# Local attention feeding a gated expert on one core: the first chunk's attention in buffers of its own, its rows of x loaded first, low parts of the weights on TensorE, loops written out, transposes a step closer

## The chip, the core and the metric

One core of one Trainium2 chip runs the program. The metric is the device time of one execution in microseconds (us), the median of several runs. A profile is one further execution, recorded by the hardware.

## What is computed

`x` is [4, 4160, 192]; `weight_gen` holds 8 heads x 7 taps per token. Each token's row is a softmax-weighted sum of the 7 rows that end at it. That goes through an expert with a hidden width of 1024, whose gate is a 3-tap convolution along the sequence:

```python
w = softmax(weight_gen, axis=-1)                     # [B, S, 8, 7]
x_unf = x_pad[:, idx, :].reshape(B, S, K, H, group)  # 7 rows that end at s
a = einsum('bshk,bskhg->bshg', w, x_unf).reshape(B, S, D)
h = maximum(a @ w_in, 0)                             # [B, S, 1024]
conv_out = sum(conv_w[k] * hp[:, k:k + S, :] for k in range(3))
gate = 1 / (1 + exp(-conv_out))
out = (h * gate) @ w_out                             # [B, S, 192]
```

## The kernel before, in words

**Chunks and steps.** The 16,640 tokens are cut into 20 chunks of 832. A chunk passes through 8 steps, one for each 128 of the 1024 hidden columns (j = 0 to 7). Every engine has its own instruction stream and runs the same sequence of steps `step(it, k)`, each with its part of the work; semaphores tie the streams together. `pipeline` writes steps 0 to 31 out, runs five rounds of a hardware loop (`Fori`) over 24 steps (three chunks, since buffers are rings of three), and writes the last 33 out.

**Attention of a chunk** (120 partitions, each with 7 tokens and the 13 rows of x they need). SyncE (SP) loads `x_win`, `logits` and `mask`. VectorE (DVE) takes maxima; GpSimd (POOL) or DVE subtracts them; ScalarE (ACT) takes exponentials; DVE sums and inverts; POOL multiplies by the inverse and by the mask into `soft` (L266, L272). Then, for i = 0 to 6: POOL multiplies the seven rows by `soft` into `weighted` (`product`, L280; a ring of three buffers, so product n waits for sum n - 3), and DVE adds up the taps into `attn` (`sum_taps`, L588). Products 2 and 5 of the first chunk are DVE's (`SHARED`). TensorE (PE) transposes `attn` in four rounds (`ROUNDS`, `turn`, L711) into the one bank `turn_ps`; ACT copies each round out as the high part (`take_turned`, L494, L496), and DVE subtracts for the low part (`low_part`, L596, L600). A round can start only when the low part of the round before has been read off the bank.

**The expert.** In each step PE multiplies the split activations by the split weights into `z` (L686, ten matmuls of 418 columns, two for each of five pairs of parts; `z` is a ring of three), two steps ahead of DVE. ACT applies relu into `hidden` (L460) and the centre tap (L467), DVE the outer taps (L558, L564), ACT the sigmoid (L478). The product with `hidden` is POOL's for six of eight steps (L417) and DVE's for j = 2 and 5 (L570). A finished output tile of 128 tokens is eight fp32 products with `wo` (L700, the trace shows each as two instructions); ACT copies it out (L503), SP stores it. A tile belongs to a step: steps 0 to 5 of the first of three chunks have one, and steps 0 to 6 of the other two; the last one or two steps of a chunk have none. The first tile is in step 32, where all of chunk 0 must be gated.

**What sets the order.** `attention_at` places the attention of chunk c at step 24 + 8c - LEAD plus a slot: maxima at -9, exponentials at -6, sums at 0 to 6, and the rounds of transposes at 4, 6, 8 and 10. LEAD is 14. POOL works two steps ahead (AHEAD) on attention, and its first chunk's products are at steps 8 to 14. In a step, PE does `product_in`, then the output tile, then `turn`.

**The start.** SP issues logits of chunks 0 and 1, the mask, x of chunk 0 (row 0 apart, then 119 partitions in one DMA, L334), the weights into `stage_a` and `stage_b` (which lie in `gated`), `wo`, and the 3072 convolution weights one by one (L386). ACT rounds the weights to their high parts (L508, L509); DVE subtracts for the low parts `wa_lo`, `wb_lo` (`weights_low`, L547), in its stream between two sums of the first chunk.

Of the kernel before, what the change touches and what calls it, by code (L numbers as in the profile page):

```python
# [11 lines left out]
P = 128  # L12
# [3 lines left out]
LEAD = 14  # L16
AHEAD = 2
LOAD = -8
LOAD_W = -10
SHARED = (2, 5)  # L20
# [28 lines left out]
def local_attention_gated_expert(nc, x, weight_gen, w_in, conv_w, w_out, masks, out):  # L49
# [18 lines left out]
    EARLY = 5  # L68
    ON_DVE = J - len(POOL_STEPS)
# [9 lines left out]
    def chunk_at(it, step):  # L79

        d, j = divmod(step, J)
        if isinstance(it, int) and not 0 <= RING * it + d < NC:
            return None
        return Chunk(it, d), j
# [8 lines left out]
    def tile_at(it, k):  # L93

        turn, step = divmod(k - J, RING * J)
# [18 lines left out]
    def products(c, i):  # L114

        first = isinstance(c.number, int) and c.number == 0
        return c.number * GROUP + i + 1 - len([n for n in SHARED if n <= i or not first])

    def attention_at(it, k, slot):

        found = chunk_at(it, k + LEAD - slot)
        return found[0] if found and found[1] == 0 else None
# [6 lines left out]
    def pipeline(eng, step):  # L129
# [3 lines left out]
        for k in range(0, 32):  # L133
            step(-1, k)
        with nc.Fori(0, 5, engines=(eng.engine,), hint_back_edge=True) as it:
            for k in range(8, 32):
                step(it, k)
        for k in range(8, 41):
            step(5, k)

    with ExitStack() as ctx:
# [43 lines left out]
        s_ident = sem("s_ident")  # L185
        s_weights_hi = sem("s_weights_hi")
# [33 lines left out]
        ROUNDS = [(4, False, 0, MID), (6, True, 0, MID), (8, False, MID, GROUP), (10, True, MID, GROUP)]  # L220
# [11 lines left out]
        def turned(i0, i1):  # L232

            return turn_ps[:, 0:(i1 - i0) * PA].rearrange("p (i c) -> p c i", c=PA)
# [5 lines left out]
        def x_landed(c):  # L240

            value = 16 * (c.turn + 1) + (16 if c.ring == 0 else 0)
# [8 lines left out]
        def shared(c, i):  # L251

            return first(c) and i in SHARED

# [19 lines left out]
        def multiply(engine, c, i):  # L274
# [4 lines left out]
            y = weighted[0:PA, (c.ring * GROUP + i) % RING, :].rearrange("p (h g k) -> p k h g", h=H, k=K)  # L279
# [10 lines left out]
        def softmax_at(it, k, slot):  # L290
# [4 lines left out]
            if c and single(c):  # L295
                return [(Chunk(0, d), 1, slice(d % RING, d % RING + 1)) for d in (c.number, c.number + 1)] \
                    if c.number % 2 == 0 else []
# [8 lines left out]
        def logits_landed(c, count):  # L306


            if single(c):
                return s_logits[c.number], 32 if c.number == 0 else 16  # L310
# [5 lines left out]
        def _(sp):  # L316
            def load(c):
                base = c.number * CHUNK
                if not isinstance(c.number, int) or c.number >= RING:

                    sp.wait_ge(s_weighted, (c.number - RING + 1) * GROUP - len(SHARED))
                    if isinstance(c.number, int) and c.number == RING:
                        sp.wait_ge(s_weighted_dve, len(SHARED))
                start = 1 if first(c) else 0
# [4 lines left out]
                if first(c):  # L329

                    sp.wait_ge(s_cleared, 2)
                    sp.dma_start(x_win[0:1, c.ring, K * D:], x_flat[0:K - 1, :].rearrange("(o a) b -> o (a b)", o=1)) \
                        .then_inc(s_x[c.ring], 16)
                sp.dma_start(x_win[start:end, c.ring, :],  # L334
                             bass.AP(x_flat.tensor, (base - K + GROUP * start) * D,
                                     [[GROUP * D, end - start], [1, WIN * D]])).then_inc(s_x[c.ring], 16)
# [7 lines left out]
            def load_logits(c, count):  # L344

                wait(sp, s_soft, c.number - (RING - 1 if single(c) else 0))
                landed = logits_landed(c, count)[0]
                for d in range(count):
                    chunk = Chunk(c.turn, c.ring + d)
                    start = 1 if first(chunk) else 0  # L350
                    end = PA - 1 if isinstance(c.number, int) and chunk.number == LAST else PA
                    if start:

                        sp.wait_ge(s_cleared, 1)
                        sp.dma_start(logits[0:1, 0, HK:], w_flat[0:GROUP - 1, :].rearrange("(o a) b -> o (a b)", o=1)) \
                            .then_inc(landed, 16)
                    sp.dma_start(logits[start:end, chunk.ring, :],
                                 bass.AP(w_flat.tensor, (chunk.number * CHUNK - 1 + GROUP * start) * HK,
                                         [[GROUP * HK, end - start], [1, GROUP * HK]])).then_inc(landed, 16)
# [7 lines left out]
            def step(it, k):  # L367
                for c, count, _ in softmax_at(it, k, LOAD_W):
                    load_logits(c, count)
                c = attention_at(it, k, LOAD)  # L370
                if c:
# [5 lines left out]

            k0 = J * RING - LEAD + J + LOAD_W
            for k in range(0, k0 + 1):
# [3 lines left out]
            sp.dma_start(stage_b[D2:P, :], w_in[P:D, :]).then_inc(s_weights, 16)  # L383
            sp.dma_start(wo[:, :, :], w_out.rearrange("(j p) d -> p j d", p=P)).then_inc(s_weights_out, 16)
            with nc.allow_non_contiguous_dma("3072 convolution weights, once"):
                sp.dma_start(cw[:, :, :], conv_w.rearrange("t (j p) -> p t j", p=P)).then_inc(s_weights_out, 16)  # L386
            for k in range(k0 + 1, 32):
                step(-1, k)
            with nc.Fori(0, 5, engines=(sp.engine,), hint_back_edge=True) as it:
# [402 lines left out]
```

## Time and profile before

| | |
|---|---|
| runs (3) | median 788.49 us, 787.89 to 789.17 |
| profiled execution | 786.22 us, span 784.4 us in the profile |
| PE busy | 701.6 us, 89% of the span |
| DVE busy | 675.3 us, 86% |
| POOL busy | 611.4 us, 78% |
| ACT busy | 523.9 us, 67% |
| granted TensorE clock, mean | 0.993 of full |
| chain that ended last | PE 81%, DVE 8%, ACT 4%, issue 3%, DMA 2% |

The span runs from the first recorded instruction to the last; the execution's own time is 1.8 us longer. "The chain" follows the last instruction back to whatever released each step. A "wait" is idle time of an engine, put down to the event that ended it.

### The profile page before, as it was taken

The page shows a single profiled execution, that of the slowest core. Times are in us where ns is not written, and L with a number is a line of the kernel's source. Part 1 is how long each engine was busy: PE and PEld are TensorE (multiplying, and loading weights), DVE is VectorE, ACT ScalarE, POOL GpSimd, SP SyncE. Part 2 cuts the span into 40 slices and gives each one's busy share as a digit, 9 for nine tenths or more (in the row PEclk, how much of TensorE's full clock was granted, in tenths as well). Part 3 has the DMA queues.
Part 4 walks back from the last instruction along what each step waited for, and adds up shares of the span by engine and source line. Part 5 has one row for each costly group of instructions (what it writes and reads, how often), then busy time and mean ns, then how long its engine had stood idle before and what let it go on. Part 6 is the DMA issues. An engine that isn't in the chain of part 4 may idle for free.

```text
span 784.4 us, 12158 instructions
## 1 busy us (share of the span) xinstructions
PE 701.6 (89%) x4008; PEld 672.9 (86%) x4008; DVE 675.3 (86%) x648; ACT 523.9 (67%) x719; POOL 611.4 (78%) x308
## 2 busy tenths in 40 slices
PE   0116698999999999989999899999999998999998
PEld 0016598999999999989999899999999998999998
DVE  3898999898999898998989998989989898985650
ACT  1117678676687676786667876678767678676761
POOL 1889999888888888998879888889878888852320
PEclk9999799999999999999999999999999999999999
DMA  7820130303323031303124030313123030000001
GB/s 155 173 54 1 30 78 16 83 21 82 78 51 72 20 82 38 91 15 83 48 50 107 21 77 20 82 41 82 42 55 79 24 90 18 20 16 21 18 26 36
DMA packets 31292, 43.11 MB, mean 55 GB/s; under 512 B 8551, under 2 KB 28614, under 8 KB 28872
## 3 DMA queue, kind: packets, MB, share of 16 engines
q1 hardware_dynamic: 31270, 42.82, 22.0%
q8 instruction: 13, 0.21, 0.1%
q14 instruction: 9, 0.07, 0.0%
HBM read 30.03 MB, written 12.78 MB: 55 GB/s over the span
## 4 chain that ended last, share of the span: by engine, by line
PE 81%; DVE 8%; ACT 4%; issue 3%; DMA 2%; POOL 1%; SPq 0%; ACTq 0%; DVEq 0%; POOLq 0%
PE out_ps L700 42%; PE z L686 34%; DVE attn L588 3%; PE turn_ps L711 3%; DMA x_win<-in_x 2%; PE z L742 2%; DVE z L558 1%; POOL weighted L280 1%; ACT hidden L460 1%; ACT L478 1%; ACT gated L478 1%; DVE z L564 1%; DVE weighted L280 1%; ACT xa_hi L496 0%; DVE wb_lo L547 0%
## 5 line engine op out<-in xcount | busy, mean ns | idle before, releaser
L280 POOL TENSOR_TENSOR weighted<-x_win,soft 120x1344 f32<-120x1344 f32 x138 | 380.7, 2768 | 55.4 <-DVE attn L588 44.2
L700 PE MATMUL out_ps<-wo,gated 128*128 128x192 f32 x2016 | 352.4, 328 | 8.1 <-ACT out_sb L503 8.1
L700 PEld LDWEIGHTS out_ps<-wo,gated 128*128 128x128 f32 x2016 | 327.6, 187 | 22.7 <-ACT out_sb L503 15.4
L417 POOL TENSOR_TENSOR gated<-gated,hidden 128x832 f32<-128x832 f32 x119 | 197.9, 1663 | 87.4 <-ACT gated L478 87.4
L588 DVE TENSOR_REDUCE attn<-weighted 120x192 f32<-120x1344 f32 x140 | 215.9, 1545 | 5.3 <-POOL weighted L280 3.3
L460 ACT ACTIVATE hidden<-z 128x836 f32<-128x836 f32 x160 | 138.7, 867 | 100.7 <-PE z L686 92.0
L558 DVE SCALAR_TENSOR_TENSOR z<-hidden,cw,z 128x832 f32<-128x832 f32 x160 | 173.1, 1082 | 16.4 <-ACT z L467 15.2
L564 DVE SCALAR_TENSOR_TENSOR z<-hidden,cw,z 128x832 f32<-128x832 f32 x160 | 174.0, 1088 | 4.3
L467 ACT ACTIVATE z<-hidden,cw 128x832 f32<-128x832 f32 x160 | 153.4, 959 | 5.2
L686 PE MATMUL z<-xa_hi,wa_hi 128*128 128x418 f32 x320 | 103.5, 405 | 20.8 <-ACT gated L478 9.3
L478 ACT ACTIVATE gated<-z 128x832 f32<-128x832 f32 x119 | 102.4, 861 | 27.0 <-DVE z L564 25.8
L711 PE MATMUL turn_ps<-ident,attn 120*128 120x120 f32 x280 | 44.1, 275 | 50.9 <-DVE attn L588 34.7
L686 PE MATMUL z<-xa_hi,wa_lo 128*128 128x418 f32 x320 | 88.3, 357 | 0.0
L686 PE MATMUL z<-xa_lo,wa_hi 128*128 128x418 f32 x320 | 88.3, 357 | 0.0
L686 PE MATMUL z<-xb,wb_hi 128*128 128x418 f32 x320 | 87.9, 356 | 0.0
L686 PE MATMUL z<-xb,wb_lo 128*128 128x418 f32 x320 | 87.8, 356 | 0.0
L711 PEld LDWEIGHTS turn_ps<-ident,attn 120*128 120x128 f32 x280 | 35.5, 146 | 55.2 <-issue 44.3
L686 PEld LDWEIGHTS z<-xa_hi,wa_hi 128*128 128x128 f32 x320 | 52.4, 192 | 26.5 <-ACT gated L478 12.8
L686 PEld LDWEIGHTS z<-xb,wb_hi 128*128 128x128 f32 x320 | 61.3, 192 | 1.0
L686 PEld LDWEIGHTS z<-xa_hi,wa_lo 128*128 128x128 f32 x320 | 61.2, 191 | 1.0
L686 PEld LDWEIGHTS z<-xa_lo,wa_hi 128*128 128x128 f32 x320 | 61.3, 192 | 0.8
L686 PEld LDWEIGHTS z<-xb,wb_lo 128*128 128x128 f32 x320 | 61.1, 191 | 0.6
(43 smaller groups left out, 378.2 us busy)
## 6 DMA issues: line engine op xcount, KB each, us to landing
x_win<-in_x SPq DMA_DIRECT2D x18, 1170.0 KB, 7.9
out<-out_sb SPq DMA_DIRECT2D x127, 96.0 KB, 1.6
logits<-in_weight_gen SPq DMA_DIRECT2D x18, 183.8 KB, 9.0
x_win<-in_x SPq DMA_DIRECT2D x2, 1160.2 KB
wo<-in_moe_w_out SPq DMA_DIRECT2D x1, 768.0 KB, 15.9
gated<-in_moe_w_in SPq DMA_DIRECT2D x1, 512.0 KB, 5.6
gated<-in_moe_w_in SPq DMA_DIRECT2D x2, 256.0 KB, 16.4
mask<-in_masks SPq DMA_DIRECT2D x20, 23.0 KB, 1.7
```

Of the source, the lines that this page charges most:

```text
L280: return engine.tensor_tensor(y, rows, s, ALU.mult)
L417: nc.gpsimd.tensor_tensor(to, to, hidden[:, (c.ring * J + j) % RING, 1:1 + CHUNK], ALU.mult) \
L460: nc.scalar.activation(hidden[:, r, :].rearrange("p (a b) -> p a b", a=2), both(r, HALF), ACT.Relu).then_inc(s_hidden, 1)
L467: nc.scalar.activation(both(r, OH), hidden[:, r, 1:1 + CHUNK].rearrange("p (a b) -> p a b", a=2), ACT.Copy, scale=cw[:, 1, j:j + 1]).then_ ...
L478: nc.scalar.activation(to, both(r, OH), ACT.Sigmoid).then_inc(s_gate, 1)
L558: nc.vector.scalar_tensor_tensor(out=both(r), in0=halves(hidden[:, r, 0:CHUNK]), scalar=cw[:, 0, j:j + 1], in1=both(r), op0=ALU.mult, op1= ...
L564: nc.vector.scalar_tensor_tensor(out=both(r), in0=halves(hidden[:, r, 2:2 + CHUNK]), scalar=cw[:, 2, j:j + 1], in1=both(r), op0=ALU.mult, ...
L588: nc.vector.tensor_reduce(attn[0:PA, i, :], y, AX.X, ALU.add).then_inc(s_attn, 1)
L686: last = nc.tensor.matmul(z[r][:, half, 0:HALF], weights, moving[:, half * HALF:(half + 1) * HALF], start=(m == 0), stop=(m == len(parts) ...
L700: last = nc.tensor.matmul(out_ps[0:end - u * P, 0:D], gated[:, j, u * P:end], wo[:, j, :], start=(j == 0), stop=(j == J - 1))
L711: last = nc.tensor.transpose(turn_ps[:, (i - i0) * PA:(i - i0 + 1) * PA], src, ident[0:PA, 0:PA])
L742: last = nc.tensor.matmul(bank[0:end - u * P, 0:D], gated[:, j, u * P:end], wo[:, j, :], start=(j == 0), stop=(j == J - 1))
```

## The change

- **First chunk.** It leaves the common sequence: SP issues `load_first`, POOL its six products, DVE `attention_first`, PE and ACT its four rounds, all before `pipeline`. Its products go to `gated[:, i, ...]`, a buffer for each i, and its rounds to four banks (`FIRST_BANKS`), so neither waits for a buffer. Only product 2 is DVE's. The maxima of chunk 1 move behind two sums.
- **Loads.** x of chunk 0 and its logits are cut into 112 and 7 partitions; x goes ahead of logits 1 to 3 and of the weights, the mask of chunk 0 behind x. The convolution weights come as 24 rows and are transposed on PE.
- **Low parts of the weights** come from PE: the staged weight times the identity, plus the high part times minus the identity, in PSUM, copied out by ACT.
- **Order.** LEAD is 13; the rounds are at slots 4, 6, 7 and 9, so rounds 3 and 4 keep their steps and all else of attention is a step later. PE does `turn` ahead of the output tile. POOL normalises the next chunk straight behind product 6.
- **Loops.** All 185 steps are written out.

The diff, cut to its core:

```diff
-LEAD = 14
+LEAD = 13
-SHARED = (2, 5)
+BY_VECTOR = 2
+    EVEN = 1 + PA // 16 * 16
-        for k in range(0, 32):
-            step(-1, k)
-        with nc.Fori(0, 5, engines=(eng.engine,), hint_back_edge=True) as it:
-            for k in range(8, 32):
-                step(it, k)
-        for k in range(8, 41):
-            step(5, k)
+        for k in range(STEPS):
+            step(-1, k)
-        ROUNDS = [(4, False, 0, MID), (6, True, 0, MID), (8, False, MID, GROUP), (10, True, MID, GROUP)]
+        ROUNDS = [(4, False, 0, MID), (6, True, 0, MID), (7, False, MID, GROUP), (9, True, MID, GROUP)]
+        FIRST_BANKS = [turn_ps, out_ps, z[2][:, 0, :], z[2][:, 1, :]]
+            y = by_hand(i) if first(c) else weighted[:, (c.ring * GROUP + i) % RING, :]
...
+            def load_first():
+                for a, b in ((1, EVEN), (EVEN, PA)):
+                    sp.dma_start(logits[a:b, 0, :], ...)
+                sp.wait_ge(s_cleared, 1)
+                sp.dma_start(logits[0:1, 0, HK:], ...)
+                for a, b in ((1, EVEN), (EVEN, PA)):
+                    sp.dma_start(x_win[a:b, 0, :], ...)
+                sp.wait_ge(s_cleared, 2)
+                sp.dma_start(x_win[0:1, 0, K * D:], ...)
+                sp.dma_start(mask[0:PA, 0, :], ...)
...
+            def normalise_next(c):
+                pool.wait_ge(s_weighted, products(c, GROUP - 1))
+                if first(c):
+                    pool.wait_ge(s_weighted_dve, 1)
+                normalise(pool, nc.gpsimd, Chunk(0, c.number + 1))
...
-            def weights_low():
-                for part, (hi, lo, stage) in enumerate(((wa_hi, wa_lo, stage_a), (wb_hi, wb_lo, stage_b))):
-                    dve.wait_ge(s_weights_hi, part + 1)
-                    nc.vector.tensor_tensor(lo[:, :], stage, hi[:, :].bitcast(F32), ALU.subtract)
+            def attention_first():
+                softmax_begin(c); sums(c); reciprocals(c); normalise(dve, nc.vector, c)
+                first_product(c, BY_VECTOR)
+                sum_taps(c, 2); sum_taps(c, 0); softmax_begin(after)
+                sum_taps(c, 1); sum_taps(c, 3); sums(after); reciprocals(after)
+                sum_taps(c, 4); low_part(c, 0); sum_taps(c, 5); low_part(c, 1)
+                sum_taps(c, 6); low_part(c, 2); low_part(c, 3)
...
+            exponent(Chunk(0, 0), 1, slice(0, 1))
+            split_weights()
+            exponent(Chunk(0, 1), 1, slice(1, 2))
+            take_conv_weights()
+            take_turned(Chunk(0, 0), 0)
+            take_rest()
+            for r in range(1, len(ROUNDS)):
+                take_turned(Chunk(0, 0), r)
...
+            def rest_of_weights():
+                pe.wait_ge(s_minus, 1)
+                for part, (hi, stage) in enumerate(((wa_hi, stage_a), (wb_hi, stage_b))):
+                    pe.wait_ge(s_weights_hi, part + 1)
+                    for half in range(2):
+                        f = slice(half * F // 2, (half + 1) * F // 2)
+                        nc.tensor.matmul(z[part][:, half, :], ident[:, :], stage[:, f], start=True, stop=False)
+                        last = nc.tensor.matmul(z[part][:, half, :], minus, hi[:, f], start=False, stop=True)
+                    last.then_inc(s_rest, 1)
```

Three places where rows stand in another order now.

**SP, from the start of its stream** (names are the tiles written and the inputs read). Before:

```order
L355 DMA logits<-in_weight_gen 1x336
L357 DMA logits<-in_weight_gen 119x392
L357 DMA logits<-in_weight_gen 120x392
L326 DMA mask<-in_masks 120x49
L332 DMA x_win<-in_x 1x1152
L334 DMA x_win<-in_x 119x2496
L381 DMA gated<-in_moe_w_in 128x1024
L382 DMA gated<-in_moe_w_in 64x1024
L383 DMA gated<-in_moe_w_in 64x1024
```

Now:

```order
L368 DMA logits<-in_weight_gen 112x392
L368 DMA logits<-in_weight_gen 7x392
L372 DMA logits<-in_weight_gen 1x336
L375 DMA x_win<-in_x 112x2496
L375 DMA x_win<-in_x 7x2496
L379 DMA x_win<-in_x 1x1152
L381 DMA mask<-in_masks 120x49
L361 DMA logits<-in_weight_gen 120x392
L404 DMA gated<-in_moe_w_in 128x1024
```

x stands ahead of the mask and of the logits of chunk 1, as 112 and 7 partitions in place of 119.

**POOL, the first two chunks** (`gated` here is the first chunk's product buffer). Before, from the product that starts chunk 0:

```order
L280 TENSOR_TENSOR weighted<-x_win,soft 120x7x192 [waits s_x0,s_soft]
L280 TENSOR_TENSOR weighted<-x_win,soft 120x7x192
L280 TENSOR_TENSOR weighted<-x_win,soft 120x7x192 [waits s_attn] x3
L266 TENSOR_TENSOR soft<-expo,inverse 120x7x8x7 [waits s_inverse,s_weighted_dve,s_weighted]
L272 TENSOR_TENSOR soft<-soft,mask 120x392 [waits s_mask1,s_norm]
L280 TENSOR_TENSOR weighted<-x_win,soft 120x7x192 [waits s_attn,s_x1,s_soft]
L280 TENSOR_TENSOR weighted<-x_win,soft 120x7x192 [waits s_attn] x6
```

Now:

```order
L295 TENSOR_TENSOR gated<-x_win,soft 120x7x192 [waits s_x0,s_soft]
L295 TENSOR_TENSOR gated<-x_win,soft 120x7x192 x5
L280 TENSOR_TENSOR soft<-expo,inverse 120x7x8x7 [waits s_inverse,s_weighted_dve,s_weighted]
L286 TENSOR_TENSOR soft<-soft,mask 120x392 [waits s_mask1,s_norm]
L295 TENSOR_TENSOR weighted<-x_win,soft 120x7x192 [waits s_x1,s_soft]
L295 TENSOR_TENSOR weighted<-x_win,soft 120x7x192 x2
L295 TENSOR_TENSOR weighted<-x_win,soft 120x7x192 [waits s_attn] x4
```

Six products stand in place of five, none of them with a wait for a sum; of chunk 1's seven, the first three have none.

**ACT, around the exponentials of three chunks**, once in 24 steps. Before (the copies to `out_sb` are the output tiles; the first one here is the fourth of its 24 steps):

```order
L503 COPY out_sb<-out_ps 128x192
L481 REGISTER_ALU
L484 ACT_TABLE_LOAD
L484 ACTIVATE expo<-logits 120x168x7
L454 REGISTER_ALU
L459 REGISTER_ALU
L460 ACTIVATE hidden<-z 128x836
L467 ACTIVATE z<-hidden,cw 128x2x416
L491 REGISTER_ALU
L494 CAST xb<-turn_ps 64x120x3
L478 ACT_TABLE_LOAD
```

Now, behind the fifth copy:

```order
L521 CAST xb<-turn_ps 64x120x3
L505 ACTIVATE z<-z 128x2x416
L530 COPY out_sb<-out_ps 128x192
L511 ACT_TABLE_LOAD
L511 ACTIVATE expo<-logits 120x168x7
L487 ACTIVATE hidden<-z 128x836
L494 ACTIVATE z<-hidden,cw 128x2x416
L505 ACT_TABLE_LOAD
```

The exponentials and the second table load moved a step later, behind the last round's copy (`xb`), to where one more tile of the chunk follows and then two steps without a tile.

## Rows read from the trace of the kernel before

**Rows 1.** Busy time by stretch: window, length, busy of PE, PEld, DVE, ACT, POOL, clock, DMA.

```profile
0.00:57.27 57.27, 3.73 (x14) 2.38 (x15) 41.66 (x41) 7.71 (x11) 33.27 (x20) 1.00 0.60 131
57.27:99.14 41.87, 29.28 (x129) 26.69 (x129) 38.86 (x39) 28.52 (x34) 39.63 (x21) 0.88 0.05 14
99.14:700.00 600.86, 587.16 (x3395) 564.86 (x3395) 552.46 (x530) 440.15 (x604) 518.61 (x257) 1.00 0.22 55
```

**Rows 2.** PE's waits from 110 to 700 us: total us, times, longest.

```profile
PE out_ps L700 <- ACT out_sb L503: 8.1, 7, 1.4
PE z L686 <- ACT gated L478: 5.6, 6, 0.9
```

**Rows 3.** The chain that ended last, at the start: start us, us, what.

```profile
2.79 15.73 DMA x_win<-in_x
...
57.27 3.43 PE z L686 x10
```

**Rows 4.** Timeline of POOL: start, us, line, out<-in, count, idle before it.

```profile
18.66 12.28 POOL L280 TENSOR_TENSOR weighted<-x_win,soft 120x1344 f32<-120x1344 f32 x4 [11.11 <-DMA x_win<-in_x]
34.67 2.65 POOL L280 TENSOR_TENSOR weighted<-x_win,soft 120x1344 f32<-120x1344 f32 x1 [3.74 <-DVE attn L588]
37.40 0.91 POOL L266 TENSOR_TENSOR soft<-expo,inverse 120x392 f32<-120x392 f32 x1
...
39.33 9.44 POOL L280 TENSOR_TENSOR weighted<-x_win,soft 120x1344 f32<-120x1344 f32 x3
51.70 10.27 POOL L280 TENSOR_TENSOR weighted<-x_win,soft 120x1344 f32<-120x1344 f32 x4 [2.93 <-DVE attn L588]
...
97.14 1.66 POOL L417 TENSOR_TENSOR gated<-gated,hidden 128x832 f32<-128x832 f32 x1 [0.84 <-ACT gated L478]
```

**Rows 5.** Loads of x, all of them: from issue to landing.

```profile
DMA to landing us min/median/max: 7.6/7.9/14.0
```

**Rows 6.** DMA traffic in two stretches; the last two columns are DMA share and GB/s.

```profile
5.00:10.00 5.00, 0.00 (x0) 0.00 (x0) 4.70 (x9) 1.06 (x2) 0.87 (x1) 1.00 1.01 218
15.40:16.80 1.40, 0.00 (x0) 0.00 (x0) 0.00 (x0) 0.00 (x0) 0.00 (x0) 1.00 0.40 125
```

**Rows 7.** Timeline of DVE at the start.

```profile
8.81 0.57 DVE L272 TENSOR_TENSOR soft<-soft,mask 120x392 f32<-120x392 f32 x1
...
18.62 2.56 DVE L280 TENSOR_TENSOR weighted<-x_win,soft 120x1344 f32<-120x1344 f32 x1 [8.17 <-DMA x_win<-in_x]
...
39.46 3.42 DVE L547 TENSOR_TENSOR wa_lo<-gated,wa_hi 128x1024 fp32r<-128x1024 f32 x1
...
47.61 1.47 DVE L259 TENSOR_TENSOR logits<-logits,top 120x392 f32<-120x392 f32 x1
```

**Rows 8.** Line L280: duration min/median/max ns, first and last start.

```profile
L280 POOL TENSOR_TENSOR weighted<-x_win,soft x138: 2587/2746/4872, 18.7 to 688.8; 120x1344 f32<-120x1344 f32 x138
```

**Rows 9.** The page's groups: busy, mean ns of one, idle before.

```profile
L417 POOL TENSOR_TENSOR gated<-gated,hidden 128x832 f32<-128x832 f32 x119 | 197.9, 1663 | 87.4 <-ACT gated L478 87.4
L460 ACT ACTIVATE hidden<-z 128x836 f32<-128x836 f32 x160 | 138.7, 867 | 100.7 <-PE z L686 92.0
...
L467 ACT ACTIVATE z<-hidden,cw 128x832 f32<-128x832 f32 x160 | 153.4, 959 | 5.2
...
L478 ACT ACTIVATE gated<-z 128x832 f32<-128x832 f32 x119 | 102.4, 861 | 27.0 <-DVE z L564 25.8
```

**Rows 10.** Timeline of PE: the first output tile, and one round of 24 steps.

```profile
99.14 2.76 PE L700 MATMUL out_ps<-wo,gated 128*128 128x192 f32 x16
...
230.43 2.87 PE L700 MATMUL out_ps<-wo,gated 128*128 128x192 f32 x16 [1.11 <-ACT out_sb L503]
...
238.46 0.65 PE L686 MATMUL z<-xa_hi,wa_hi 128*128 128x418 f32 x2 [0.94 <-ACT gated L478]
```

**Rows 11.** Timeline of ACT in the same round.

```profile
223.12 1.28 ACT L484 ACT_TABLE_LOAD   x1
224.41 1.19 ACT L484 ACTIVATE expo<-logits 120x1176 f32<-120x1176 f32 x1
```

More of the change, by code:

```diff
@@ L114, in products @@
     def products(c, i):
-        first = isinstance(c.number, int) and c.number == 0
-        return c.number * GROUP + i + 1 - len([n for n in SHARED if n <= i or not first])
+        return c.number * GROUP + i + 1 - (1 if c.number > 0 or i >= BY_VECTOR else 0)
     def attention_at(it, k, slot):
-        found = chunk_at(it, k + LEAD - slot)
-        return found[0] if found and found[1] == 0 else None
+        for c in range(1, NC):
+            if k == J * RING + c * J - LEAD + STALL + slot:
+                return Chunk(0, c)
+        return None
     def wait(eng, sem, value):
@@ L319, in load @@
                 if not isinstance(c.number, int) or c.number >= RING:
[L321 to L324, printed above, removed]
+                    sp.wait_ge(s_weighted, products(Chunk(0, c.number - RING), GROUP - 1))
+                    if c.number == RING:
+                        sp.wait_ge(s_weighted_dve, 1)
                 end = PA - 1 if isinstance(c.number, int) and c.number == LAST else PA
@@ L368, in step @@
                 for c, count, _ in softmax_at(it, k, LOAD_W):
-                    load_logits(c, count)
+                    if not single(c):
+                        load_logits(c, count)
                 c = attention_at(it, k, LOAD)
-                if c:
+                if c and c.number >= RING:
                     load(c)
@@ L375, in step @@
                     store(*found)
-            k0 = J * RING - LEAD + J + LOAD_W
-            for k in range(0, k0 + 1):
-                step(-1, k)
+            load_first()
+            load_logits(Chunk(0, 1), 1)
             sp.dma_start(stage_a, w_in[0:P, :]).then_inc(s_weights, 16)
@@ L383, in _ @@
             sp.dma_start(stage_b[D2:P, :], w_in[P:D, :]).then_inc(s_weights, 16)
+            sp.dma_start(conv_rows, conv_w.rearrange("t (j p) -> (t j) p", p=P)).then_inc(s_conv_rows, 16)
+            load_logits(Chunk(0, 2), 1)
+            load_logits(Chunk(0, 3), 1)
+            load(Chunk(0, 1))
             sp.dma_start(wo[:, :, :], w_out.rearrange("(j p) d -> p j d", p=P)).then_inc(s_weights_out, 16)
[L385 to L389, printed above, removed]
-                for k in range(8, 32):
-                    step(it, k)
-            for k in range(8, 41):
-                step(5, k)
+            load(Chunk(0, 2))
+            pipeline(step)
             for turn, u in last_tiles():
@@ L442, in step @@
                     apply_gate(*found)
-            pipeline(pool, step)
+            for i in range(GROUP):
+                if i != BY_VECTOR:
+                    product(Chunk(0, 0), i)
+            normalise_next(Chunk(0, 0))
+            pipeline(step)
         @block.scalar
```

204 lines of the change are left out of this document (127 added, 77 removed).

## The prediction

> **What bounds the kernel now.** I read the stretches first. From 99.14 us, where the first output tile starts, to 700 us PE is busy 587.2 of 600.9 us, DVE 552.5, POOL 518.6 [rows 1]. So from the first tile on PE alone sets the time, and the end is the start of that tile plus 784.4 - 99.1 = 685.3 us. Ahead of it PE did little: 3.7 of 57.3 us, then 29.3 of 41.9. PE's waits give the rest: 13.7 us from 110 to 700, all of it for ACT (8.1 for copies of output tiles, 5.6 for sigmoids), and none without a named cause [rows 2]. The chain of waits shows what held the start: 15.7 us for x of chunk 0, and z of chunk 0 only at 57.27 [rows 3]. The timeline of POOL then shows a nearly full engine up to the last gate of chunk 0 at 98.8 us, 0.3 us ahead of the first tile [rows 4, 10]. So the change is worth what it takes off POOL's chain up to that gate, plus what it does to the 13.7 us.
>
> **Part 1: when the first product starts.** Before, x was issued at 2.79 and landed at 18.52 [rows 3]; product 0 started at 18.66 [rows 4]. In the last of that transfer only 0.40 of the DMA engines' time was used, at 125 GB/s; from 5 to 10 us it was all of it, at 218 [rows 6]. The 120-partition loads of x land in 7.6 to 7.9 us, the largest value being 14.0 [rows 5]. So 119 partitions are the odd case, not the size.
>
> The Trainium skill (DMA: Bandwidth & Descriptors, "Why a DMA increments its semaphore by 16 and not by 1") says that a DMA is spread over the largest number of engines, up to 16, that divides its outer dimension: 119 gives 7, 112 gives 16. The share of 0.40 agrees (7/16 is 0.44). By the rule 112 partitions go in seven rounds where 120 take eight on 15, so x would land an eighth sooner than 7.6 us, about 1 us less than what I take.
>
> Now x is issued behind three DMAs of logits, at some 2.0 us. At the landing time of a 120-partition load it would be there at 9.6 to 9.9; the seven partitions, row 0 and the mask come behind it in the same queue. I take 10.6 for the last of them, and DVE's multiplication by the mask, 0.57 us [rows 7], which used to be done long ahead and now waits for it. The first product starts at **11.2**. Low bound 10.2 (nothing behind x costs anything), high bound 16.6 (14.0 us for x).
>
> **Part 2: POOL's chain to the last gate of chunk 0.** Product 0 starts together with DVE's product, as before, and takes the longest time of the line, 4.87 us, which is DVE's 2.56 and then its own [rows 7, 8]. Five more have no wait and no other two-operand work of DVE beside most of them: 2.6 each (shortest 2.587 [rows 8]), to 11.2 + 4.9 + 13.0 = 29.1. Normalising chunk 1 takes from 37.40 to 39.33, 1.9 [rows 4]: 31.0. Seven products of chunk 1 at 10.27/4 = 2.57 [rows 4]: 49.0. Chunk 2 is normalised: 50.9. Then seven products of chunk 2 at the median 2.75 [rows 8], another normalisation and six gates at 1.66 [rows 9]: 19.2 + 1.9 + 10.0, to 82.0. Before, the stretch from 61.97 to 98.80 held the same and one product more, which LEAD 13 moves behind the gate: 35.8 of work in 36.8, so 1.0 idle. I keep it: 83.0.
>
> What went, against 18.66: POOL's two waits for a sum, 3.74 and 2.93 [rows 4], which came of the ring of three buffers and of the low parts in DVE's stream (3.42 and its twin [rows 7]); 0.5 us on each of three products beside these (9.44/3 against 2.57 [rows 4]); one product. What came: one product for POOL in place of DVE (2.6, counted).
>
> What could be late next is DVE and PE. The low parts on PE are four fp32 and four split matmuls of 512 columns. Eight fp32 products of 192 columns take 2.76 us at the full clock [rows 10], so 512 columns cost about 0.9, or 1.8 at 1.2 GHz; a split matmul of 418 columns took 0.34 us when z of chunk 0 came out of a pause [rows 3], so 512 cost 0.42. That is 4 x 2.2 = 8.9 us at the low clock. It starts when the weights are in and rounded: 1 MB behind x at 218 GB/s [rows 6] is 16, with the first cast some 17.5 us. PE is free between 24 and 26.4, where round 1 of the transposes could start at about 23.5 (fourth sum); ACT then copies both low parts ahead of round 2. DVE ends the last low part at 33.6 to 35.4, does the maxima and subtractions of chunks 2 and 3 (each subtraction 0.6 to 1.5 [rows 7]) and the first sum of chunk 1 by 38.4 to 40.5. POOL's fourth product of chunk 1 needs that sum and is due at 31.0 + 7.7 = 38.7. So 0 to 2 us of wait; I take 1. The gate ends at 84.0, the first tile starts at **84.3** against 99.14: **14.8 us** less.
>
> The Trainium skill (SBUF — State Buffer, "SBUF: two separate sides") says that DVE with two SBUF inputs and POOL exclude each other for a whole instruction. The rows above agree (4.87 is one behind the other). By the rule each of DVE's three subtractions in this stretch could wait out a whole product, 2.6 us, where the row of this trace shows 1.47 in place of about 0.6; the wait of POOL would then be 4 us, not 1.
>
> From the taps on DVE is close behind POOL as before: between first tap and first tile it has seven sums, eight pairs of taps, and one low part more than it had (0.66). It stays some 2 us ahead of the last gate by my count, so it costs nothing; if POOL is faster than I think, DVE is the next bound, at about 82.
>
> **Part 3: from the first tile on.** PE's work is the same. The loops' back edges go; PE had no unexplained idle [rows 2], so this is worth 0. POOL enters with one product less done (2.7 us), at 518.6/600.9 = 86% load [rows 1]; the first chunk with tiles may stall for part of it: **+1**.
>
> The ACT waits: once in 24 steps ACT loads a table, takes exponentials (1.28 + 1.19 [rows 11]) and loads a table again; PE then waits 1.11 + 0.94 = 2.05 us [rows 10], first for the copy of a tile, then for a sigmoid. The exponentials now come one step later, behind one more tile copy and the copy of the last transposes. By the timeline of that round: PE finishes the next tile without waiting, since the copy ahead of it is done; then come the two steps without a tile, where z needs sigmoids one and two steps back. The next tile's copy would be done at some 227.8; table and exponentials end at 230.3; relu 0.87, centre tap 0.96, table 1.28 and sigmoid 0.86 [rows 9, 11] give the first sigmoid at 234.3, and copy, relu, tap and sigmoid the next at 237.3. PE, with a tile and two z between, would ask at 233.7 and 236.6: 1.3 us in place of 2.05. Over six to seven rounds that is nearly 5; I take **-3**, since DVE may be late for a sigmoid. Bounds: all of the 13.7 us goes, or each round pays 2.05 more, +12.
>
> Rounds 1 to 2 and 2 to 3 of the transposes are now two and one steps apart. Round 3 needs DVE's low part of round 2, issued in the same step. PE spends some 4.5 us in a step with a tile; from the end of z to that low part I count 7.4 us over two such steps, against 9.4 until PE asks for it. It costs nothing as long as the margin of 2 us holds. All else that moves (SP's loads, turns ahead of tiles) keeps its distance.
>
> **Sum.** -14.8 + 1 - 3 = **-16.8 us**. The profiled execution took 786.22 (span 784.4 and 1.8 around it): 769.4. It lay 2.27 below the median of the runs, so the median becomes 788.49 - 16.8 = **771.7 us**.
>
> **The rivals.**
> 1. *The start is later than that* (chance 0.2): x lands late, PE runs the low parts at the low clock throughout, and DVE's subtractions wait out whole products, so POOL waits 4 or more. For: nothing of this overlap was in the trace. Against: POOL's chain was tight before too. 2 to 8 us more: 774 to 780.
> 2. *ACT's waits all but vanish* (0.13): the step without a tile absorbs the table loads. For: they were only 2.05 a round. Against: my timeline still finds two. 7 to 10 us less than the forecast, 762 to 765.
> 3. *Slower* (0.03): the rounds bind. If round 3 waits w us for the low part of round 2 in every chunk after the first, it costs 19w. The gain of 16.8 is gone from w = 0.9; at w = 2 the time is 788.5 - 16.8 + 38 = 810. For: DVE is at 92% [rows 1], so it fills 4.1 of the 4.5 us of a step. Against: the 2 us of margin above.
> 4. *It doesn't do what it says* (0.04): PE gets its first tile 15 us sooner but DVE, not PE, sets the pace for the rest, so the lead is paid back: 786 to 789. Against: DVE's 92% [rows 1] leaves 48 us of slack.
>
> The forecast itself has 0.60. **The range** is 762 to 780: it takes in rivals 1 and 2 for the greater part, and the bounds on the first product (-1, +5) and on ACT. A difference of 0.2% is 1.6 us, about what a measurement of this kernel can tell from none. **Faster 0.95, same 0.01, slower 0.04** (rival 3 and a share of rival 4).
>
> **What would show it.** In the profile after: first product of POOL near 11 us; its chunk 0 products in one piece of about 18 us without a wait; z of chunk 0 near 34 to 36; first tap near 46; first tile near 84; PE's waits for ACT after that 9 to 11 us in all, with none for transposes. A first tile after 88, a total of waits above 16, or a row of PE waiting for L640 or L644 in each chunk would make the prediction wrong.

## The result, and the profile after

The changed kernel takes **766.61 us** (median of 4 runs, 765.41 to 767.54) against 788.19 for the kernel before on the same chip (786.99 to 789.17): a ratio of 0.9729, 95% interval 0.9709 to 0.9749, or 21.6 us less. I had forecast 16.8 less. It is inside the range, but the parts do not fall where I put them. The profiled execution took 767.54 us with a span of 765.8, 18.7 less than that of the kernel before (786.22), which lay at the low end of its runs while this one lies at the high end. (Two of the four executions took 765.4 and 765.8 us, two 767.4 and 767.5; the profiled one is the longest.)

The page of the changed kernel, busy time and the slices of PE:

```profile
PE 707.7 (92%) x4021; PEld 681.8 (89%) x4021; DVE 666.6 (87%) x646; ACT 526.1 (69%) x723; POOL 610.6 (80%) x308
...
PE   1655899999999999999999999999999999999998
```

Busy time by stretch, columns as in [rows 1]; the cuts are the first z of chunk 0 and the first output tile:

```profile
0.00:33.11 33.11, 9.26 (x28) 5.33 (x28) 23.09 (x31) 8.84 (x13) 22.56 (x15) 0.93 0.92 211
33.11:86.04 52.93, 32.43 (x128) 28.82 (x129) 49.84 (x45) 29.45 (x35) 47.81 (x25) 0.79 0.08 20
86.04:700.00 613.96, 603.19 (x3501) 586.65 (x3502) 565.55 (x544) 454.21 (x626) 526.92 (x262) 1.00 0.22 55
```

The first z starts at 33.11 and the first tile at 86.04, against 57.27 and 99.14 [rows 1, 3]: of the 24 us won at z, 11 are gone by the first tile, since DVE and POOL need 52.9 us for what lies between, where they needed 41.9 with more of chunk 1 already done. From the first tile to the end the span is 765.8 - 86.04 = 679.8 us, against 685.3. So 13.1 us came ahead of the first tile and 5.5 behind it.

The start, on POOL, DVE and PE, in that order. The rows answer to [rows 4, 7, 10]:

```profile
11.02 17.70 POOL L295 TENSOR_TENSOR gated<-x_win,soft 120x1344 f32<-120x1344 f32 x6 [9.55 <-DVE soft L286]
...
30.73 8.02 POOL L295 TENSOR_TENSOR weighted<-x_win,soft 120x1344 f32<-120x1344 f32 x3
40.58 10.20 POOL L295 TENSOR_TENSOR weighted<-x_win,soft 120x1344 f32<-120x1344 f32 x4 [1.83 <-DVE attn L631]
```

```profile
10.37 0.57 DVE L286 TENSOR_TENSOR soft<-soft,mask 120x392 f32<-120x392 f32 x1 [3.24 <-DMA mask<-in_masks]
...
33.59 2.60 DVE L273 TENSOR_TENSOR logits<-logits,top 120x392 f32<-120x392 f32 x1
36.11 0.55 DVE L650 TENSOR_REDUCE top<-logits 120x56 f32<-120x392 f32 x1
36.69 2.34 DVE L273 TENSOR_TENSOR logits<-logits,top 120x392 f32<-120x392 f32 x1
```

```profile
23.58 0.57 PE L776 MATMUL turn_ps<-ident,attn 120*128 120x120 f32 x4
...
86.04 4.52 PE L763 MATMUL out_ps<-wo,gated 128*128 128x192 f32 x16 [2.04 <-POOL gated L445]
```

Product 0 starts at 11.02 (forecast 11.2), the six products take 17.70 us in one piece (17.9), and POOL waits once, 1.83 us, for the first sum of chunk 1. That sum is late because each of DVE's two subtractions took about as long as a product of POOL. PE waited 2.04 us for POOL's last gate, and then ran its first tile in 4.52 us in place of 2.76; the granted clock of the stretch is 0.71:

```profile
86.04:92.00 5.96, 5.96 (x25) 5.94 (x26) 5.22 (x6) 4.28 (x7) 5.96 (x3) 0.71 0.04 12
```

PE's waits from 110 to 700 us answer to [rows 2] (`issue` stands where the profile names nothing that ended the wait):

```profile
PE out_ps L763 <- issue: 6.1, 6, 1.6
PE z L749 <- ACT gated L505: 4.6, 11, 0.7
```

They sum to 10.7 us against 13.7. In a period of 24 steps they are 0.3 us shorter (1.78 against 2.05 [rows 10]), yet the period takes 105.3 us (the tile that waits starts at 122.62, 227.89, 333.18) where it took 106.2 (124.17, 230.43, 336.64). A part of what was won behind the first tile stands in no wait at all. That was the question for the experiments, beside what each part of the start is worth.

### The profile page after: what moved, and what is told of

It reads as the page before. It is cut to its first block, busy times and chain, and to the rows that moved or that the text cites. A ratio compares the mean times of both kernels' runs of the same rounds, so it can differ in the third digit from the quotient of the medians.

```text
span 765.8 us, 10644 instructions
## 1 busy us (share of the span) xinstructions
PE 707.7 (92%) x4021; PEld 681.8 (89%) x4021; DVE 666.6 (87%) x646; ACT 526.1 (69%) x723; POOL 610.6 (80%) x308
## 4 chain that ended last, share of the span: by engine, by line
PE 78%; ACT 9%; POOL 5%; issue 4%; DVE 3%; DMA 1%; SPq 0%; DVEq 0%; POOLq 0%; ACTq 0%
PE out_ps L763 39%; PE z L749 33%; PE turn_ps L776 3%; ACT hidden L487 2%; POOL gated L295 2%; PE z L805 2%; POOL weighted L295 2%; ACT gated L505 1%; DVE attn L631 1%; ACT L505 1%; ACT L511 1%; ACT z L494 1%; DMA mask<-in_masks 1%; ACT expo L511 1%; POOL gated L445 1%
## 5 line engine op out<-in xcount | busy, mean ns | idle before, releaser
L295 POOL TENSOR_TENSOR weighted<-x_win,soft 120x1344 f32<-120x1344 f32 x133 | 365.3, 2752 | 75.8 <-DVE attn L631 75.6
L631 DVE TENSOR_REDUCE attn<-weighted 120x192 f32<-120x1344 f32 x133 | 205.3, 1545 | 0.0
L749 PE MATMUL z<-xa_hi,wa_hi 128*128 128x418 f32 x320 | 108.8, 422 | 15.4 <-ACT gated L505 8.4
L749 PEld LDWEIGHTS z<-xa_hi,wa_hi 128*128 128x128 f32 x320 | 55.7, 194 | 22.6 <-ACT gated L505 14.6
L776 PE MATMUL turn_ps<-ident,attn 120*128 120x120 f32 x270 | 41.1, 269 | 9.0 <-DVE attn L631 5.4
L640 DVE TENSOR_TENSOR xb<-turn_ps,xb 64x480 fp32r<-64x480 f32 (+1 forms) x38 | 22.8, 601 | 28.7 <-ACT xb L521 27.8
```

The costliest lines, as they stand in the source:

```text
L295: return engine.tensor_tensor(y, rows, s, ALU.mult)
L631: nc.vector.tensor_reduce(attn[0:PA, i, :], y[0:PA].rearrange("p (d k) -> p d k", k=K), AX.X, ALU.add) \
L640: nc.vector.tensor_tensor(columns(xb[D2:P, c.ring, :], i0, i1), src[D2:P], columns(xb[0:D2, c.ring, :].bitcast(F32), i0, i1), ALU.subtract ...
L749: last = nc.tensor.matmul(z[r][:, half, 0:HALF], weights, moving[:, half * HALF:(half + 1) * HALF], start=(m == 0), stop=(m == len(parts) ...
L776: last = nc.tensor.transpose(bank[:, (i - i0) * PA:(i - i0 + 1) * PA], src, ident[0:PA, 0:PA])
```

## The experiments

All are timed over three rounds against the kernel before on the same chip. "Changed" is the changed kernel, 766.6 us. The variants ran on different chips, where the kernel before took 786.8 to 788.2 us, so a difference of about 1 us between two variants says little.

### Loops written out, alone

```diff
-        with nc.Fori(0, 5, engines=(eng.engine,), hint_back_edge=True) as it:
+        for it in range(5):
```

in the kernel before, SP's loop the same.

> The kernel before with its five rounds of the loop written out and nothing else. In the two profiles a round of 24 steps takes 106.2 us before and 105.3 after, but PE's named waits in it differ by only 0.2 us (2.02 against 1.80). Theory L (loops): the other 0.7 us is the loop's own (the back edge and the register work between instructions), so this kernel gains 0.7 us in each of six rounds: 4 to 5 us, 783 to 784, with a round of 105.5. Theory O (order): it is the order of transposes and tiles, and this kernel stays at 788, with a round of 106.2.

788.39 us against 787.55, ratio 1.0007 (0.9996 to 1.0019): **no gain**. That the jumps of the loop cost time is out. Two small effects nearly cancel in the profile. PE's last wait of 1.43 us in the kernel before, for a tile copy just behind the last round of the loop (672.16 us), is gone; but a step that follows transposes takes 4.70 to 4.76 us in place of 4.63 to 4.68, and a period 106.6 in place of 106.2. Why is open.

### PE's transposes ahead of the tile, alone

```diff
+                for r, (slot, *_) in enumerate(ROUNDS):
+                    ... turn(c, r)
                 found = tile_at(it, k)
                 if found:
                     product_out(*found)
-                for r, (slot, *_) in enumerate(ROUNDS):
-                    ... turn(c, r)
```

in the kernel before.

> The kernel before with one edit: in a step PE does its round of transposes ahead of the output tile, not behind it. Theory C (the copy of a tile is queued on ACT behind the copy of the round): before, the round ends a step, ACT takes it out, does a sigmoid and only then copies the tile, 1.9 us after the round, which is when PE has finished z and wants the bank; steps that follow a round take 4.63 to 4.76 us in place of 4.50. With the round first this goes: a round of 24 steps takes 105.1 us in place of 106.2, 6 to 7 us in all: 781. Rival (the changed kernel's shorter rounds come from something else, the loads or the first chunk): no change, 788.

**779.41 us against 787.07**, ratio 0.9911 (0.9894 to 0.9927): 7.7 us less for one exchange of lines. Here is one step of each kernel. First PE and ACT of the kernel before:

```profile
240.47 2.77 PE L700 MATMUL out_ps<-wo,gated 128*128 128x192 f32 x16
...
243.08 0.58 PE L711 MATMUL turn_ps<-ident,attn 120*128 120x120 f32 x4
...
245.47 2.87 PE L700 MATMUL out_ps<-wo,gated 128*128 128x192 f32 x16
```

```profile
243.69 0.63 ACT L494 CAST xb<-turn_ps 64x480 fp32r<-64x480 f32 x1 [0.55 <-PE turn_ps L711]
244.34 0.88 ACT L478 ACTIVATE gated<-z 128x832 f32<-128x832 f32 x1
245.11 0.31 ACT L503 COPY out_sb<-out_ps 128x192 f32<-128x192 f32 x1
```

and of turnfirst:

```profile
238.45 0.57 PE L711 MATMUL turn_ps<-ident,attn 120*128 120x120 f32 x4
...
238.87 2.77 PE L700 MATMUL out_ps<-wo,gated 128*128 128x192 f32 x16
...
243.39 2.76 PE L700 MATMUL out_ps<-wo,gated 128*128 128x192 f32 x16
```

```profile
241.14 0.64 ACT L494 CAST xb<-turn_ps 64x480 fp32r<-64x480 f32 x1
242.08 0.87 ACT L478 ACTIVATE gated<-z 128x832 f32<-128x832 f32 x1 [0.30 <-DVE z L564]
242.84 0.32 ACT L503 COPY out_sb<-out_ps 128x192 f32<-128x192 f32 x1
```

Before, the transposes end the step. ACT stands idle until 243.69 for them, copies, does a sigmoid, and copies the tile only at 245.11 to 245.42, though the tile was done at 243.2. PE, which has spent 1.9 us on z meanwhile, gets the bank at 245.47. With the transposes first, the tile's copy ends at 243.16, 0.23 ahead of PE. The step that follows, from z at 243.41 (241.34 in turnfirst) to the next z, takes 4.63 us before and 4.52 here. The pause is 0.1 to 0.2 us, below what the profile lists as a wait (a matmul's end is modelled and covers it). In this period it comes in five of the eight tile steps that follow a round (4.63 to 4.67 us against 4.50 to 4.52).

A period takes 105.0 us here, 1.2 less. Of these, steps behind a round give 0.5 and listed waits 0.2, which fits the copy. But a step that holds both a round and a tile is also shorter, mostly 4.80 to 4.84 us in place of 4.84 to 4.89, which makes 0.4 over nine steps; no copy of a tile is late in it that the rows show, and its cause is open. So the order of the two is what counts, by experiment; that ACT's queue is the reason is shown for about half of it.

### LEAD and the rounds back to 14

```diff
-LEAD = 13
+LEAD = 14
-        ROUNDS = [(4, False, 0, MID), (6, True, 0, MID), (7, False, MID, GROUP), (9, True, MID, GROUP)]
+        ROUNDS = [(4, False, 0, MID), (6, True, 0, MID), (8, False, MID, GROUP), (10, True, MID, GROUP)]
```

> The changed kernel with LEAD 14 and the rounds of transposes at slots 4, 6, 8 and 10 as before; first chunk, loads and written-out steps stay. Theory A (exponentials a step later save little): PE's waits go from 1.8 back to about 2.0 us a round, 1 to 1.5 us in all, and POOL has one product more ahead of the last gate of chunk 0, which moves the first tile by up to 2.7 us: 768 to 770.5. Theory O (the order of attention gave the gain behind the first tile): a round goes back to 106.2 us and the time up by 5 us or more, 772.

**764.76 us**, 0.9712 (0.9695 to 0.9728), 1.9 less than the changed kernel: neither expectation held, since both said more. How much less is not sharp, because the two intervals overlap and the two executions of the changed kernel at 765.4 and 765.8 are only 0.6 to 1.0 longer. "A step closer" is no gain, and probably a small loss. The first tile comes later, at 87.14, but PE does not wait for POOL's gate there and runs it at the full clock (2.77 us). PE's waits behind it are as long in all (10.6 us against 10.7), and a period is 105.1 against 105.3:

```profile
PE z L749 <- ACT gated L505: 5.5, 6, 0.9
PE out_ps L763 <- ACT out_sb L530: 5.1, 6, 1.0
```

The waits are as long, but they are not the same ones. With LEAD 13 the wait for the copy behind the exponentials is gone, as forecast. In its place PE waits at the first tile of the next three chunks, which the profile puts down to `issue`. POOL and PE of the changed kernel there:

```profile
224.52 3.27 POOL L445 TENSOR_TENSOR gated<-gated,hidden 128x832 f32<-128x832 f32 x2
```

```profile
227.89 2.84 PE L763 MATMUL out_ps<-wo,gated 128*128 128x192 f32 x16 [0.88 <-issue]
```

POOL's last gate of the chunk ends at 227.79 and the tile, whose instructions stand behind a wait for that gate in the code, starts 0.10 later. The same 0.10 lies between gate and tile at all six of these waits (the first is 122.52 and 122.62). With LEAD 14 the same gate ends at 226.24 and the tile starts at 226.98 without a wait. So LEAD 13 took one wait off ACT and put one as long on POOL.

### The start alone

The changed kernel with LEAD 14 as above, and PE's transposes behind the tile.

> The changed kernel with LEAD 14, rounds at slots 4, 6, 8, 10 and PE's transposes behind the tile as before: of the change only the start and the written-out steps are left. Theory (the parts add up): the first tile comes at 87.1 as in lead14, and from there it takes the 685.3 us of the kernel before, since the transposes again hold the copies back: 12.0 us less than the kernel before, 774 to 775.5, and PE's order is worth 9 to 10 us in the changed kernel. Rival (PE's order is worth the 7.6 us that turnfirst showed and something else of the change shortens the stretch behind the first tile): 772 to 773.

**774.14 us** against 787.79, ratio 0.9831 (0.9815 to 0.9847). The parts add up: first tile at 86.69, and 772.6 - 86.7 = 685.9 us from there, close to the 685.3 of the kernel before. By the medians the start is worth 13.7 us; PE's order, from here to lead14, is worth 9.4; LEAD 13 costs 1.9 (less surely, as said above); together 21.2 of the measured 21.6. That the order is worth more here than the 7.7 of turnfirst has its place in the period: with the old order it is 106.2 us in the kernel with the loop and 106.6 to 106.7 with the steps written out (unroll and here), and with the transposes first it is 105.0 and 105.1.

### x of chunk 0 in one DMA

```diff
-                for a, b in ((1, EVEN), (EVEN, PA)):
+                for a, b in ((1, PA),):
                     sp.dma_start(x_win[a:b, 0, :], ...)
```

> The changed kernel with rows 1 to 119 of the first chunk's windows in one DMA of 119 partitions in place of 112 and 7. Theory S (spread of the transfer): x takes 15.7 us again, from an issue at 1.9, so it lands at 17.6, the mask behind it, and the first product starts at about 18.3 in place of 11.0. POOL's chain moves with it: 7 us more, 773.5. Rival (the start is bound by DVE and PE by now, or the order of the loads was what mattered): 2 us or less, 768.5.

**774.16 us**, 0.9822 (0.9803 to 0.9841): 7.6 more than the changed kernel. The first product moves from 11.02 to 17.61 and all else with it:

```profile
17.61 17.68 POOL L295 TENSOR_TENSOR gated<-x_win,soft 120x1344 f32<-120x1344 f32 x6 [16.14 <-DVE soft L286]
```

About half of what the start is worth is the cut of 119 partitions into 112 and 7.

### Low parts of the weights on DVE

```diff
                 low_part(c, 0)
+                weights_low()
                 sum_taps(c, 5)
```

with the matmuls and ACT's two copies for them taken out.

> The changed kernel with the low parts of the weights subtracted on DVE again (two instructions of 3.4 us, behind the first low part of the first chunk); no matmuls and no copies by ACT for them. Theory D (DVE's stream is on the path): the last low part of chunk 0, the four softmax instructions and the first sum of chunk 1 come 5 to 7 us later, POOL's fourth product of chunk 1 waits for it, and the first tile comes 4 to 6 us later: 771 to 773. Rival (POOL's own work hides it, since its wait there is only 1.8 us): 1 us or less, 767.5.

**769.40 us**, 0.977 (0.9753 to 0.9786): 2.8 more, between the two. The two subtractions take 4.9 us of DVE in place of 6.9, since one of them fell between products. POOL's wait for the first sum of chunk 1 rises to 2.90, the six products take 18.52 in place of 17.70, and the first tile starts at 88.33, 2.3 later.

### First products in the ring; one bank for the first transposes

ring: products in `weighted`, waits from product 3 on, sums in the order 0 to 3. onebank: `FIRST_BANKS = [turn_ps] * 4`, each round waiting for `s_lo`.

> The changed kernel with the first chunk's products in the ring of three buffers again, each product from 3 on waiting for the sum three before it (sums in the order 0, 1, 2, 3). Theory R (own buffers are worth little once only product 2 is DVE's): a sum takes 1.55 us where a product takes 2.6, so POOL waits only where the softmax of chunk 1 stands between sums: 0 to 1.5 us, 767 to 768. Rival (the buffers gave the 3.7 us wait that went): 3 us or more, 770.

> The changed kernel with all four rounds of the first chunk's transposes in the one bank again, each waiting for the low part before it. Theory B (own banks are worth the last round only): rounds 1 and 2 have time, since the sums set them; round 4 waits for low part 3, so the last low part of chunk 0 comes about 1 us later. DVE's next work is blocked by POOL's products anyway (2.60 and 2.34 us), so the first tile comes 0 to 1 us later: 766.6 to 767.6. Rival: 2.5 us or more, 769, since every round's chain of transposes, copy and subtraction adds up.

ring **766.53 us** (765.59 to 767.59), onebank **765.56** (765.35 to 767.06): neither buffers nor banks of its own are worth anything that these runs can tell. In ring POOL's products take 17.69 us in one piece. In onebank the last low part comes at 34.2 in place of 33.0, but the first of the two subtractions then takes 1.07 us in place of 2.60, because, as I read it, it no longer has a whole product ahead of it. The ring alone does not bring back the wait of 3.74 us [rows 4]. In the kernel before, the sum that POOL waited for stood behind DVE's second product:

```profile
29.18 4.05 DVE L280 TENSOR_TENSOR weighted<-x_win,soft 120x1344 f32<-120x1344 f32 x1
```

So the wait probably went with that product; no run gives it back to DVE.

### Maxima of chunks 2 and 3 in PSUM

```diff
+        def top_of(c, part):
+            if c.number in (2, 3):
+                return out_ps[0:PA, 64 * (c.number - 2):64 * (c.number - 2) + GROUP * H]
+            return top[0:PA, part, :].rearrange("p n a -> p (n a)")
```

> The changed kernel with the maxima of chunks 2 and 3 in a free PSUM bank, so that DVE's two subtractions have one operand in SBUF and one in PSUM. Theory P (two SBUF operands shut DVE out while POOL runs a product): the subtractions took 2.60 and 2.34 us; they take 0.6 now, the first sum of chunk 1 starts at 35.1 in place of 38.96, POOL's wait of 1.8 us before its fourth product goes, and the first tile comes 1.8 us sooner: 764.8. Rival (DVE is slowed by something else, or the later chain is bound by taps and reliefs nothing): the subtractions stay above 2 us, or the time stays at 766.6.

**763.38 us**, 0.9703 (0.9686 to 0.9719): 3.2 less than the changed kernel. DVE and POOL:

```profile
33.46 0.56 DVE L279 TENSOR_TENSOR logits<-logits,out_ps 120x392 f32<-120x392 f32 x1
33.94 0.56 DVE L656 TENSOR_REDUCE out_ps<-logits 120x56 f32<-120x392 f32 x1
34.54 0.56 DVE L279 TENSOR_TENSOR logits<-logits,out_ps 120x392 f32<-120x392 f32 x1
```

```profile
30.72 17.88 POOL L301 TENSOR_TENSOR weighted<-x_win,soft 120x1344 f32<-120x1344 f32 x7
```

The same subtraction takes 0.56 us where it took 2.60 and 2.34, beside the same products of POOL. Only the place of one operand differs. The Trainium skill (SBUF — State Buffer, "SBUF: two separate sides") names that: a DVE instruction with two SBUF inputs and a GpSimd instruction that reads SBUF shut each other out for a whole instruction. Here the trace agrees. The first tile moves by 2.1 us, to 83.91. The rest of the 3.2 goes with the first tile itself: PE waits 1.72 us ahead of it in place of 2.04 and runs it in 2.84 us at the full clock. Against the two executions of the changed kernel at 765.4 and 765.8 the gain is 2.0 to 2.4 us.

### A version from these, and two steps further

best is lead14 with psumtop and the mask of chunk 0 ahead of x.

> The changed kernel with LEAD 14 and rounds at slots 4, 6, 8, 10; the maxima of chunks 2 and 3 in PSUM; and the mask of chunk 0 issued ahead of x. From lead14 (764.8): the first product starts when x is there and not 0.6 to 1.0 us later, and POOL's wait of 1.8 us goes. If POOL's chain sets the first tile: 762. If DVE's taps do: 763.5 to 764.5.

**762.23 us** (762.04 to 762.41), 0.9688 (0.9672 to 0.9704), first tile at 84.81. POOL starts at 10.59 and now waits for x itself, so the mask cost 0.4 us.

copyfirst is best with one exchange on ACT:

```diff
+                behind = k > J * (RING + 1) and softmax_at(it, k - 1, -6)
+                if found and behind:
+                    take_out(*found)
```

> Kernel best (762.2), with ACT's copy of the output tile ahead of the sigmoid in the one step of 24 that follows the exponentials. Theory: PE's wait of 0.95 us for that copy, 5.1 us over six rounds, is the copy standing behind a table load and a sigmoid (1.28 + 0.86 us); it goes, and the wait of 0.92 for the sigmoid stays: 757 to 758, with a round of 104.1 in place of 105.1. Rival: the sigmoid, 0.3 us later, sets PE's next wait, and what is won on the tile is lost on z: 761 to 762.5.

**762.09 us** (761.81 to 762.14): the same within the noise. The wait of the tile behind the exponentials goes, and one of nearly the same length opens two steps behind the sigmoid's:

```profile
221.17 0.65 PE L759 MATMUL z<-xa_hi,wa_hi 128*128 128x418 f32 x2 [0.92 <-ACT gated L511]
...
229.17 2.84 PE L773 MATMUL out_ps<-wo,gated 128*128 128x192 f32 x16 [0.86 <-ACT out_sb L536]
```

The period is 105.0 again. PE can be only so far ahead of ACT, and ACT's 3.8 us of table loads and exponentials must be made up somewhere; moving the place moved the wait. (That it must be so is my reading; the trace shows the one wait gone and the other opened.)

gatefirst is best with POOL's gate ahead of its product up to the first tile.

> Kernel best (762.2), with POOL's gate ahead of its product in each step up to the first tile. Theory G (ACT's relu waits for POOL's first gates, and DVE for ACT, ahead of the first tile): relu starts 2.6 us sooner there, DVE's taps with it, and the first tile comes 1 to 2.5 us sooner: 760 to 761. Rival (DVE's own stream is full, or POOL now waits for ACT's sigmoids with products behind it): no gain or a loss of up to 2 us, 762 to 764.

**763.19 us** (762.40 to 764.45). The first tile comes 1.4 us sooner, at 83.38, and PE gives it back at the third tile after it:

```profile
99.42 2.84 PE L773 MATMUL out_ps<-wo,gated 128*128 128x192 f32 x16 [2.05 <-ACT out_sb L540]
```

There POOL is a product behind, ACT's relu at 96.02 waits 3.6 us for its gate (1.3 in best), and the copy of the tile stands behind that relu. A first tile that is sooner than POOL can follow is no gain.

## Why the prediction was right, and where it was not

- **What bounds the kernel: held.** PE from the first tile on; startonly shows the stretch behind it untouched to 0.6 us while the start moved by 12.5.
- **When the first product starts: right** (11.2 forecast, 11.02 measured). That the mask would be last held too: it landed at 10.3 (10.6 forecast). Onex shows the price of 119 partitions (6.6 us on the first product, 7.6 in all).
- **POOL's chain: right in its pieces** (17.9 against 17.70; wait 1 against 1.83), late by 1.7 us at the end: first tile 86.04 in place of 84.3 (z of chunk 0 came at 33.11, sooner than forecast, the first tap at 47.38, later). What I had under-sized is DVE's two subtractions, which I priced at 0.6 to 1.5 each from the old trace and which took 2.60 and 2.34. The rule that I quoted beside them gave 2.6 for each of three, and the measurement sides with it for these two; the first of the three took 0.72, and POOL's wait was 1.83, not the 4 that I had worked out by the rule. Psumtop shows that this delay is the operands' place, worth 2 to 3 us in all.
- **What went: partly wrong.** I put POOL's 3.74 us wait down to the ring of three. Ring shows that the ring does not matter once DVE has one product, not two.
- **"-3" for the exponentials a step later: wrong.** The named waits did fall by 3.0 us (13.7 to 10.7, in the 9 to 11 that I gave), but that is luck: they are 10.6 with LEAD 14. I had foreseen that the wait for the copy would go. I had not looked at POOL's last gate of a chunk, for which PE then waited 0.9 us at the first tile behind; 6.1 of the 10.7 us are waits for it and not for ACT, as I had said they would be. LEAD 13 gained nothing and may have cost up to 1.9 us. copyfirst shows a like thing on ACT: a wait taken from one tile comes back at a later one. Of the "+1" for a stall of POOL behind the first tile nothing shows: PE has no listed wait from there to 110 us.
- **"All else that moves (SP's loads, turns ahead of tiles) keeps its distance": this is the step that failed.** I costed PE's new order at nothing; it is worth 7.7 us in the old kernel and 9.4 in the new. I had taken the 13.7 us of named waits for all that PE loses behind the first tile, and looked for the price of the order only in whether transposes wait for low parts. About half of the loss is seen on ACT, where a tile's copy queued behind the copy of transposes that PE had put last; a part in the steps with both is not explained.
- **Loops: right at 0**, by unroll.
- **The low clock: missing.** PE's 2.04 us pause ahead of the first tile was followed by 4.52 us for the tile; in kernels that paused 1.62 to 1.83 us there (dvelow, psumtop, onebank) it took 2.84. The length of the pause is not the whole of it: in gatefirst a later tile took 2.84 us behind a pause of 2.05, with a granted clock of 1.00 (99.42 to 102). What differs is what PE had done before: 16 us of work in a row with no listed wait there, while in the changed kernel PE had stood for 4.39 us up to 75.46 and then run at a mean granted clock of 0.56 up to 79.3. Which of these decides, no run tells. I had the clock in the price of the low parts alone, where it hardly mattered: their matmuls held the first round of transposes from 22.75, when its last sum ended, to 23.58, but DVE had sums to do until 25.2.
- The forecast of -16.8 for the -21.6 measured came out as near as it did by luck, because errors of both signs met: 1.7 us too much at the first tile, 4 to 5 too much for LEAD, and the order of PE, up to 9.4, not counted at all.

## What to carry to other kernels

When one engine's stream feeds another that serves several of its results in a fixed order, try issuing first what the consumer takes first, even where the producer is the bound and shows no wait (7.7 to 9.4 us here): compare the time from one step's start to the next, not only the listed idle. Where a wait is listed without a releaser, look for what ended just before it on every engine. Moving a long piece of work on the consumer moved the wait twice here and did not remove it, so test such a move before crediting it. And look at a load's partition count before its size: 119 partitions took 15.7 us, 112 and 7 under 8.4.

## What the runs showed of the hardware that I had not expected

A subtraction on VectorE of 120x392 elements took 0.56 us with one operand in PSUM and, with both in SBUF, 2.34 to 2.60 us beside GpSimd's products of 2.6 us (1.07 in onebank, where it was issued later, and 0.57 in dvelow, where GpSimd stood still). A tile of eight fp32 products took 2.77 us, 2.84 behind a pause of 1.6 to 1.8 us, and 4.52 behind one of 2.04 (after and ring; onex with 2.08), with a granted clock of 0.71 over the next 6 us; yet 2.84 behind one of 2.05 in gatefirst. TensorE lost 0.1 to 0.25 us in each of several steps per period that no listed wait shows (4.63 to 4.76 us in place of 4.50 to 4.52 in before, unroll and startonly).
